# Expert stage of an attention and mixture-of-experts kernel: the second weight in eight-row runs per partition, the first weight read by every eighth column

## The reference

```python
def _moe_ref(x, expert_emb, tau, w1, w2) -> np.ndarray:
    ...
    for e in range(E):
        mask = expert_idx == e
        if not mask.any():
            continue
        h = np.maximum(x[mask] @ w1[e], 0.0)
        out[mask] = gate_w[mask, None] * (h @ w2[e])
    return out.astype(np.float32)

def reference(**kwargs):
    ...
    attn_out = _attn_ref(**attn_kwargs)
    B, H, S, D = attn_out.shape
    x = np.ascontiguousarray(attn_out.transpose(0, 2, 1, 3)).reshape(B * S, H * D)
    x = _moe_ref(x=x, **moe_kwargs)
    return _moe2_ref(x=x, **moe2_kwargs)
```

## Time and profile before

| | |
|---|---|
| median of 3 runs | 1176.4 us (1176.33 to 1177.39) |
| the profiled execution, its own time | 1178.32 us |
| its span | 1176.5 us |
| PE busy | 1102.0 us, 94% of the span |
| weight loads (PEld) busy | 1007.7 us, 86% |
| DVE, ACT, POOL busy | 56%, 47%, 32% |
| mean granted clock of TensorE | 0.979 |
| expert stage, first product to last slot's end | 435.4 to 747.9 us |

### The profile page before, as it was taken

One profiled execution on the slowest core, in us unless ns is written; L12 is line 12 of the kernel. 1 busy time (PEld: TensorE's weight loads), 2 busy tenths in 40 slices (PEclk: granted clock), 3 DMA queues, 4 the chain that ended last, 5 costly groups with the idle time before them and its releaser, 6 DMA issues. The chain is left out here.

```text
span 1176.5 us, 25336 instructions
## 1 busy us (share of the span) xinstructions
PE 1102.0 (94%) x10424; PEld 1007.7 (86%) x10424; DVE 658.3 (56%) x1315; ACT 551.5 (47%) x1137; POOL 382.3 (32%) x329
## 2 busy tenths in 40 slices
PE   2799999999999989999999999599999999999998
PEld 1488888888887879999999999489999999999997
DVE  4588888888788626665555555353434334343332
ACT  2467777777676634544444444143333323233322
POOL 3566667777776622113333420320100100000000
PEclk9999999999999969999999999799999999999999
DMA  7112223333232059999979830230100100000000
GB/s 112 21 29 36 43 49 69 76 83 75 57 82 50 15 195 396 392 392 391 389 274 391 285 117 28 85 90 1 54 1 28 28 4 24 1 28 1 28 1 27
DMA packets 131875, 130.75 MB, mean 111 GB/s; under 512 B 78440, under 2 KB 118576, under 8 KB 131760
## 3 DMA queue, kind: packets, MB, share of 16 engines
q1 hardware_dynamic: 122176, 107.30, 29.1%
q0 software_dynamic: 5120, 15.73, 4.0%
q10 hardware_dynamic: 4464, 6.10, 1.4%
HBM read 129.70 MB, written 21.43 MB: 128 GB/s over the span
## 5 line engine op out<-in xcount | busy, mean ns | idle before, releaser
L1577 PE MATMUL mlp_ps<-xg_t,win 128*128 128x512 f32 x864 | 215.6, 396 | 1.4 <-DVE xg_t L1659 1.4
L1577 PEld LDWEIGHTS mlp_ps<-xg_t,win 128*128 128x128 f32 x864 | 161.2, 189 | 31.9 <-DVE xg_t L1659 1.8
L1240 PE MATMUL expert_ps<-xs_t,w_sb 128*128 128x128 f32 x1488 | 174.0, 278 | 0.6 <-ACT xs_t L1270 0.6
L1240 PEld LDWEIGHTS expert_ps<-xs_t,w_sb 128*128 128x128 f32 x1488 | 173.0, 194 | 1.4 <-ACT xs_t L1270 1.0
L1666 DVE TENSOR_TENSOR sq<-relu 128x512 f32<-128x512 f32 x96 | 66.6, 694 | 157.9 <-ACT relu L1618 156.3
L1322 DVE TENSOR_TENSOR w_hl<-w_sb,w_hl 128x1536 fp32r<-128x1536 f32 x62 | 110.1, 1777 | 71.6 <-ACT w_hl L1279 71.5
L1251 PE MATMUL expert_ps<-w_hl,ht_hl 128*128 128x384 f32 x744 | 137.6, 340 | 0.2 <-issue 0.2
L767 DVE TENSOR_TENSOR p_cur<-newt,cst 128x256 f16<-128x256 f32 x288 | 108.8, 419 | 50.2 <-PE newt L413 47.0
L1618 ACT ACTIVATE relu<-mlp_ps 128x512 f32<-128x512 f32 x96 | 57.4, 598 | 168.3 <-PE mlp_ps L1577 167.9
L1251 PEld LDWEIGHTS expert_ps<-w_hl,ht_hl 128*128 128x128 f32 x744 | 128.5, 188 | 0.4 <-issue 0.4
L1279 ACT CAST w_hl<-w_sb 128x1536 fp32r<-128x1536 f32 x62 | 91.3, 1476 | 60.6 <-PE expert_ps L1251 60.6
(11 more groups left out here) (205 smaller groups left out, 1803.7 us busy)
## 6 DMA issues: line engine op xcount, KB each, us to landing
w_sb<-in_moe_w SPq DMA_DIRECT2D x62, 1536.0 KB
xs<-sorted_x SPq DMA_DIRECT2D x31, 192.0 KB, 11.2
sorted_y<-ys ACTq DMA_DIRECT2D x31, 192.0 KB, 5.9
k_raw<-in_k SPq DMA_DIRECT2D x24, 192.0 KB, 3.0
q_pad<-in_q SPq DMA_DIRECT2D x24, 192.0 KB, 3.8
v_raw<-in_v SPq DMA_DIRECT2D x24, 192.0 KB, 4.1
out<-o_sb SPq DMA_DIRECT2D x6, 768.0 KB, 3.5
sorted_x<-zeros SPq DMA_DIRECT2D x11, 384.0 KB, 5.5
```

The costliest lines, as they stand in the source:

```text
L1240: mm = pe.matmul(ps[:, 1 + half, c * P:(c + 1) * P], w1_sb[j % 2][:, kd, f], xs_t[:, kd], start=(kd == 0), stop=(kd == KD - 1))
L1577: mm = pe.matmul(ps[:, 4 + f % 2, :], win[:, a, kd, f * P:(f + 1) * P], xg_t[:, par, b, kd], start=(kd == 0 and a + b == 0), stop=(kd == K ...
```

## The change

Row `r` of `w2` now lies on partition `r // 8` in block `r % 8`, where it lay on partition `r % 128` in block `r // 128`. A partition's part of `w2` in memory becomes one run of 8 x 384 floats (12,288 bytes) instead of eight runs of 384 floats (1,536 bytes). To fit, block `c` of the first product takes the columns `c, c + 8, c + 16, ...` of `w1`: the 128 floats that LDWEIGHTS reads in a partition lie 32 bytes apart instead of 4. `w1` itself is loaded as before.

```diff
     def load_w2(self, sp, w2, e, u, cond=None):
-        sp.dma_start(self.w2_sb[u][:, :, :], w2[bass.ds(e, 1)].rearrange("o (k p) d -> p (o k) d", p=P), cond=cond)\
+        sp.dma_start(self.w2_sb[u][:, :, :], w2[bass.ds(e, 1)].rearrange("o (p k) d -> p (o k) d", p=P), cond=cond)\
           .then_inc(self.s_w2[u], 16)
...
                 for c in range(HK):
-                    f = slice((HK * half + c) * P, (HK * half + c + 1) * P)
                     for kd in range(KD):
-                        mm = pe.matmul(ps[:, 1 + half, c * P:(c + 1) * P], w1_sb[j % 2][:, kd, f], xs_t[:, kd],
+                        rows = w1_sb[j % 2][:, kd].rearrange("p (t k) -> p k t", k=K1)[:, HK * half + c]
+                        mm = pe.matmul(ps[:, 1 + half, c * P:(c + 1) * P], rows, xs_t[:, kd],
                                        start=(kd == 0), stop=(kd == KD - 1))
```

## The result

The change makes the kernel 15% slower: 1358.9 us (median of 4 runs, 1357.0 to 1359.7) against 1176.9 us; the ratio is 1.1541, with a 95% interval of 1.1521 to 1.1561. My forecast was no change, at 1176.4 us, and my range ended at 1342 us. All medians and ratios here are of undisturbed executions; one execution of a later kernel (the one with the runs only), at 1256.2 us with a mean granted clock of 0.844, is left out of its ratio.

A forecast was written before the change was run, and what follows sets the result against it. TensorE's own pace was taken to bound the kernel. Load of w2 0, first product 0, the rest untouched: span 1176.5 us, profiled execution 1178.3, less 1.9 to the median gives 1176.4 us; range 1174 to 1342.

The forecast's parts named there:

- what bounds the kernel: Expert stage, slots 1 to 30: TensorE's own pace is the bound, 9.88 us a slot, almost without waits.
- the transfer: Load of w2: a faster one could give at most 0.2 us, at slot 2; booked at 0.
- no cover: First product: the float32 weight load is not hidden behind its matmul; any added length is paid 1,488 times.
- If a jump to a far address costs one more such step, this load has the step free: First product's weight load: it asks 1.15 floats in a ns, half the 2.2 shown in the dense layer; booked at 0.
- the lower end: First product: the stepped weight load costs nothing extra, 111.5 ns a pair stay; chosen for the forecast.
- the bound from above: First product: a load with twice the steps, 221 ns a pair, 5.26 us a slot, 163 us in 31 slots.
- the right rival: First product: the weight load takes twice the steps, uncovered; +163 us, 1339 us; chance 0.27.
- In between: First product: jumps partly hidden, or the load meets transfers' writes more often; +82 us, 1258 us; chance 0.14.
- Slower transfer: Load of w2 in long runs is slower; at half pace at most 98 us more, 1275 us; chance 0.05.
- a gain by a faster one: Shorter w2 transfer gives more than slot 2's 0.2 us; faster by over 0.2% had chance 0.05.
- Clock: First product: longer loads leave the array less busy and the granted clock falls; +492 us; chance 0.02.
- Contention with the transfers' writes: First product: the stepped load meets transfers' writes in SBUF more often; part of the +82 us case, chance 0.14.

The follow-up runs named there:

- the runs-only kernel: Only w2 loaded in one run of 12,288 bytes a partition, weight loads adjacent as in the kernel before: 1176.1 us against 1176.5, ratio 1.0003.
- The dense layer's kernel: Kernel before, but weight loads of the dense layer's first product read every 8th column of win: 1194.4 us, ratio 1.016.
- by twos: Kernel before, but the 512 moving columns of the dense layer's first product are read with a step of two columns: 1365.0 us, ratio 1.1596.
- step 2: Kernel before with a step of 2 columns (8 bytes) in the first product's weight loads, w2 in runs of two rows: 1184.0 us, ratio 1.007.
- step 3: Kernel before with a step of 3 columns (12 bytes) in the first product's weight loads, blocks overlapping: 1265.3 us (one run).
- the moving operand at step 8: Kernel before with adjacent weight loads, but the first product's moving operand xs_t read with a step of 8 columns: 1355.3 us (one run).

## Why the prediction was wrong

**Right: what bounds the kernel, and the transfer.** TensorE's pace sets the expert stage and the w2 transfer sets nothing; the runs-only kernel shows this within 0.15%. The packets fell to 110,371, where I had about 110,400, and 110,371 - 107,184 = 3,187 are over 8 KB, 3,072 more than the 115 of before: 24 loads of 128 runs, each run one packet.

**Right: no cover.** I wrote that the load alone sets the pace of the pair, so that what it gains in length is paid 1,488 times. It gained 125 ns and was paid so, but for slot 0, where it gained 24 ns as long as the clock was at half. The dense layer's kernel shows the other side: with a matmul of 512 columns beside it the stepped load costs 19 ns.

**Wrong: the step that failed.** It is the sentence "If a jump to a far address costs one more such step, this load has the step free", with the choice of the lower end that rests on it. I compared floats in a ns: 1.15 asked for, 2.2 shown in the dense layer. The measure that counts is pieces of 16 bytes in a ns. The dense stream of adjacent columns opens 128 pieces in 228 ns, 0.56 in a ns, and the runs show that this is the limit itself: by twos, with 256 pieces, it takes 453 ns, twice as long. The load with adjacent columns opens 32 in 111.5 ns and has room for twice that, which is why step 2 is nearly free. With step 8 it asks for 128 in 111.5 ns, 1.15 in a ns, twice the limit. The same row that I read as spare room showed a stream with none.

**Wrong: the bound from above.** Twice the steps of the array was priced at 221 ns a pair from slot 0 at half clock, +163 us. The price is not in steps of the array: in slot 0 of the changed kernel a pair takes 238 ns at half clock and at full. It is a time of about 1.8 ns for each piece read, and 128 pieces are 236 ns, 15 ns over my bound. In 30 slots that is 22 us, and slot 0 gives some of it back, since its pairs took over 210 ns already at half clock. So the range ended 17 us under the result even with the right rival. What in the reading takes the 1.8 ns, no run shows. My 221 ns was also read a little high: it is a mean over the first 26 pairs, of which the first alone took 0.37 us (435.36 to 435.73) and the others 214 ns each. The mechanism of this rival, a load that takes about twice as long with nothing to cover it, was right in kind, and it had 0.27.

**The other rivals.** In between: not for step 8, but it is what step 3 does. Slower transfer, and a gain by a faster one: excluded by the runs-only kernel. Clock: the granted clock was 1.00 in slots 1 to 29, so it did not fall, with loads of twice the length. Contention with the transfers' writes: the pace is the same at a DMA share of 0.04.

No experiment points to a version faster than the kernel before: the long runs give nothing where transfers are hidden, and every step of the load from 2 columns on costs.

## What to carry to other kernels

Before an operand of TensorE is read with a step, count the pieces of 16 bytes that a load or a matmul opens in a partition, and multiply by 1.8 ns (1.7 to 1.85 in these runs, all with operands of 4 bytes). If that is more than its time with adjacent columns at the clock that is granted, it takes that long instead. For a load the price is hidden only as far as a longer matmul runs beside it. A layout that makes a transfer's runs longer is worth nothing where no engine waits for the transfer, so what it costs on the reading side is a pure loss. And where two streams are compared to see whether one has room, compare them in the unit in which the memory is read.

## What the runs showed of the hardware

- Both operands of TensorE pay the same price for opened pieces: 1.85 ns in the weight load and 1.82 ns in the moving operand at step 8.
- This price does not follow TensorE's clock: 238 ns a pair at half clock and at full, while the load of adjacent columns took 214 and 111.5. Where the columns need longer than the pieces, the step is free: step 3 took 213 ns at half clock, 172 at full.
- A matmul of 512 adjacent columns of the dense layer's kind stands at this limit already at the full clock (228 ns), and not at half clock (426 ns).
- The two operands do not share the limit: 128 pieces of a load and 128 of a matmul took 247 ns together.
- Runs of 12,288 bytes to a partition went as one packet each, and a transfer in such runs neither shortened nor lengthened a slot.
